# Attention and two MLPs on one core: four matmuls on constants at the outset, and transfers at other places in the queues

## The reference

```python
def _attn_ref(q, k, v, tau):          # q, k, v: (2, 6016, 256), float32
    qn = q / (np.linalg.norm(q, axis=1, keepdims=True) + 1e-06)
    kn = k / (np.linalg.norm(k, axis=1, keepdims=True) + 1e-06)
    s = kn.transpose(0, 2, 1) @ qn / tau          # (2, 256, 256)
    s = s - s.max(-1, keepdims=True)
    a = np.exp(s)
    a /= a.sum(-1, keepdims=True) + 1e-09
    return v @ a

def _moe_ref(x, w_gate, w_val, w_out):            # x: (12032, 256), d_ff 1536
    gate = 1.0 / (1.0 + np.exp(-(x @ w_gate)))
    return gate * (x @ w_val) @ w_out

def _moe2_ref(x, w_in, w_out):                    # d_ff 2048
    h = x @ w_in
    return (h - np.tanh(h)) @ w_out

# reference: _moe2_ref(_moe_ref(_attn_ref(...)))
```

## Time and profile before

| | |
|---|---|
| time, median of 3 runs | 2216.34 us |
| the profiled execution's own time | 2216.27 us |
| its span | 2214.4 us |
| PE busy | 2192.7 us, 99% |
| PEld busy | 1908.6 us, 86% |
| DVE busy | 1547.5 us, 70% |
| ACT busy | 1276.4 us, 58% |
| POOL busy | 1157.3 us, 52% |
| DMA | 439.46 MB, 198 GB/s over the span |

### The profile page before, as it was taken

How to read it: one execution, slowest core, us unless ns; L and a number is a source line. 1 busy time by engine, 2 the same in 40 slices (tenths; PEclk the granted TensorE clock), 3 DMA queues, 4 the chain that set the end, 5 groups by cost and what they waited for, 6 DMA issues and landing times.

```text
span 2214.4 us, 33619 instructions
## 1 busy us (share of the span) xinstructions
PE 2192.7 (99%) x11664; PEld 1908.6 (86%) x11664; DVE 1547.5 (70%) x2933; ACT 1276.4 (58%) x2336; POOL 1157.3 (52%) x970
## 2 busy tenths in 40 slices
PE   8999999999999999999999999999999999999998
PEld 7878988888888898898998898888888888889998
DVE  6868866866776685686586586586586577567566
ACT  5644654665565565565565465465466456556555
POOL 3476663564465474365364365356356446446434
PEclk9999999999999999999999999999999999999999
DMA  9997476376367357447557546537536546635644
GB/s 340 341 298 271 154 225 221 134 228 213 140 214 235 132 175 225 178 169 241 188 197 227 188 166 207 188 134 221 190 126 213 183 141 200 203 126 183 232 143 150
DMA packets 286473, 439.46 MB, mean 198 GB/s; under 512 B 208096, under 2 KB 214496, under 8 KB 286304
## 3 DMA queue, kind: packets, MB, share of 16 engines
q1 hardware_dynamic: 279184, 409.82, 56.3%
q0 software_dynamic: 5264, 27.27, 3.3%
q10 hardware_dynamic: 1856, 0.23, 0.1%
HBM read 386.14 MB, written 51.12 MB: 197 GB/s over the span
## 4 chain that ended last, share of the span: by engine, by line
PE 91%; DMA 3%; SPq 2%; DVE 2%; issue 1%; ACT 1%; POOL 0%; ACTq 0%; DVEq 0%; POOLq 0%
PE up L1595 52%; PE x_acc L1595 20%; PE acc L1595 18%; DMA qk_in<-in_k 1%; DMA w_stage<-in_moe_w_out 1%; PE x_acc L1621 1%; SPq L410 1%; SPq L486 1%; DMA u_records<-x_lo 1%; SPq L488 0%; DVE sq_sum L1187 0%; SPq L399 0%; ACT up L832 0%; DMA ring<-u_records 0%; DVE g_lo L1311 0%
## 5 line engine op out<-in xcount | busy, mean ns | idle before, releaser
L735 POOL TENSOR_TENSOR g<-t_sums,g 128x512 fp32r<-128x512 f32 (+1 forms) x384 | 503.1, 1327 | 375.6 <-ACT g L1022 375.4
L725 POOL TENSOR_TENSOR g_lo<-func_out,g_hi 128x512 fp32r<-128x512 f32 (+1 forms) x253 | 314.2, 1271 | 571.7 <-ACT g_hi L957 571.4
L1595 PE MATMUL up<-vt_hi,ring 128*128 128x512 f32 (+1 forms) x1848 | 562.4, 385 | 0.0
L1595 PEld LDWEIGHTS up<-vt_hi,ring 128*128 128x128 f32 x1848 | 347.1, 188 | 63.0
L1595 PE MATMUL up<-vt_lo,ring 128*128 128x512 f32 (+1 forms) x924 | 358.7, 388 | 1.5 <-DMA ring<-u_records 1.3
L1324 DVE TENSOR_TENSOR held<-up,held 128x512 f32<-128x512 f32 (+1 forms) x132 | 89.7, 680 | 367.9 <-PE up L1595 367.9
L1022 ACT ACTIVATE g<-t_sums 128x512 fp32r<-128x512 f32 (+1 forms) x384 | 237.9, 619 | 160.1 <-DVE t_sums L1407 159.7
L1595 PE MATMUL x_acc<-g,ring 128*128 128x256 f32 (+1 forms) x2304 | 304.4, 281 | 0.0
L1595 PE MATMUL up<-x_lo,in_w_hi 128*128 128x512 f32 (+1 forms) x768 | 298.0, 388 | 0.0
L1595 PE MATMUL up<-x_hi,in_w_lo 128*128 128x512 f32 (+1 forms) x768 | 297.4, 387 | 0.0
L1595 PE MATMUL up<-x_hi,in_w_hi 128*128 128x512 f32 (+1 forms) x768 | 295.9, 385 | 0.0
(11 more groups left out here) (257 smaller groups left out, 3621.8 us busy)
## 6 DMA issues: line engine op xcount, KB each, us to landing
...
ring<-u_records SPq DMA_DIRECT2D x132, 896.0 KB, 6.0
...
```

Source lines behind the costliest of these rows:

```text
L725: pool.tensor_tensor(g1_lo[:, i, 0:w], func_out[:, i, 0:w], g1_hi[:, i, 0:w].bitcast(F32), ALU.subtract).then_inc(g_lo_made, 2 if last and ...
L735: pool.tensor_tensor(lo[:, cut, 0:half], t_sums[:, first - T1:first - T1 + 2, 0:half], hi[:, cut, 0:half].bitcast(F32), ALU.subtract).then ...
L1595: mm = pe.matmul(psum, a, b, start=start and n == 0, stop=stop and n == 2, skip_group_check=shared_bank)
```

## The change

It has eight parts. (1) PE makes four matmuls of the constant `ones` with itself, into a bank that is written anew later, before its first gram chunk. (2) POOL loads pieces 0 and 1 of the weights when 8 gram chunks are done (before: 2), piece 2 at 12 (before: 4) and piece 3 at 14 (before: 7), and it is piece 2 whose split waits for the attention weights of batch 0 (before: piece 4). (3) The eight parts of v for unit 0 are loaded with the last four chunks of batch 0, two with each (before: with the chunks 4 to 11, one with each); DVE turns them and DVE and ACT split them two chunks of batch 1 later, and the second unit's come behind batch 1's chunks. (4) SP waits for all of q and k to have landed before it saves the first raw part. (5) Of the folded parts only the first three pieces' are stored ahead of the first sums; the others follow one by one behind each of the first three sums. (6) In ACT's `first_chunk`, `first_hi` comes ahead of `hi_of_u_sums`. (7) The outputs of a tile's unit 0 are stored in the next tile's `body`, behind its first two ring records and two d records. (8) The last four products are given in two steps, and DVE's last sums begin behind the first of them and turn the first half before the rest.

```diff
@@ -310,7 +310,7 @@
         p_hi_made, p_lo_made = sem("p_hi_made"), sem("p_lo_made")
         t_sums_made, t_hi_made, t_lo_made = sem("t_sums_made"), sem("t_hi_made"), sem("t_lo_made")
         o_made, m_copied, out_summed = sem("o_made"), sem("m_copied"), sem("out_summed")
-        last_three_made = sem("last_three_made")
+        last_three_made, last_two_made = sem("last_three_made"), sem("last_two_made")
         out_turned, stored = sem("out_turned"), sem("stored")
 
         block = ctx.enter_context(nc.Block())
@@ -364,9 +364,9 @@
             return 16 + 16 * STORES * (n + 1)
 
         TURN_ATT = 12
-        EARLY_PIECES = 4
-        V_TURN, V_SPLIT = 12, 13
-        SECOND_V_TURN, SECOND_V_SPLIT = 10, 11
+        WARM_UP = 4
+        EARLY_PIECES, PIECES_AT = 2, [8, 8, 12, 14]
+        V_TURN, V_SPLIT = 14, 15
         EARLY_FOLDS = 3
         FOLD_AT, FOLD_SUMS_AT = 1, 2
 
@@ -436,10 +436,13 @@
                         sp.dma_start(qk_in[:, buf, which, ahead:size, :],
                                      rows[:, bass.ds(block0, size - ahead), :]
                                      ).then_inc(qk_loaded[buf], 16)
-                    if r in (1, 2):
-                        if b == 1 and r == 1 and buf == 0:
+                    if b == 0 and r == ROUNDS - 1:
+                        for part in (2 * buf, 2 * buf + 1):
+                            load_v_part(0, 0, 0, W, part)
+                    if b == 1 and r in (1, 2):
+                        if r == 1 and buf == 0:
                             sp.wait_ge(v_turned, 1)
-                        load_v_part(0, 0, b, W, (r - 1) * BUFS + buf)
+                        load_v_part(0, 0, 1, W, (r - 1) * BUFS + buf)
 
             def save_raw(n):
                 sp.wait_ge(w_split, n + 1)
@@ -536,7 +539,6 @@
                             sp.wait_ge(fold_stored[n], 32)
                     load_ring(NEXT_G, u_records[b_next, record(0, 0)])
                 load_o(t, BOTH - 1)
-                store(t, b, 0, w)
 
             def body(t, b, w, w_before, b_before, nxt, b_next, fold=False):
                 sp.wait_ge(o_made, BOTH * (t - 1) + BOTH - 2)
@@ -545,6 +547,7 @@
                 load_gate(t, b, 1)
                 for p in range(2):
                     load_d(t, p)
+                store(t - 1, b_before, 0, w_before)
                 if fold:
                     sp.wait_ge(p_made, 2 * BOTH * t)
                     load_raw(t - 1)
@@ -580,12 +583,13 @@
             for b in range(B):
                 for r in range(1 if b == 0 else 0, ROUNDS):
                     load_qk(b, r)
+            sp.wait_ge(qk_loaded[BUFS - 1], 32 * B * ROUNDS)
             for n in range(FOLDS):
                 save_raw(n)
             for n in range(J1 // 4):
                 store_d(n)
             load_v(1, 0, 0, W)
-            for n in range(FOLDS):
+            for n in range(FOLDS // 2):
                 store_a_parts(n)
             load_d(0, 2, first=True)
             for n in range(FOLDS):
@@ -594,6 +598,8 @@
                     load_d(0, 2 + (n + 1) // 2, first=True)
                 if n == 1:
                     load_v(1, 0, 1, W)
+                if n < FOLDS // 2:
+                    store_a_parts(FOLDS // 2 + n)
             sp.wait_ge(u_a_stored, 16 * 8 * FOLDS)
             sp.wait_ge(first_up_made, 4 * J1)
             rest_of_tile(0, 0, W, W, 0, first=True)
@@ -606,6 +612,7 @@
                 body(t, 1, W, W, 1, W, 1)
             body(TILES - 2, 1, W, W, 1, W_END, 1)
             body(TILES - 1, 1, W_END, W, 1, None, 1)
+            store(TILES - 1, 1, 0, W_END)
             store(TILES - 1, 1, 1, W_END)
             sp.wait_ge(stored, all_stored(LAST_SUB))
 
@@ -628,8 +635,8 @@
 
             def load_next(n):
                 if n + 2 < PIECES:
-                    if n + 2 < EARLY_PIECES:
-                        pool.wait_ge(gram_made, 4 + 3 * n)
+                    if n + 2 < len(PIECES_AT):
+                        pool.wait_ge(gram_made, PIECES_AT[n + 2])
                     elif SECOND_BLOCK <= n + 2:
                         pool.wait_ge(gram_made, B * CHUNKS - 6)
                     pool.wait_ge(w_split, n + 1)
@@ -789,7 +796,7 @@
                         lo_of_fold_sums(t - 1)
                 both_subs(t, w, nxt)
 
-            pool.wait_ge(gram_made, 2)
+            pool.wait_ge(gram_made, PIECES_AT[0])
             load(0)
             load(1)
             for n in range(WHOLE):
@@ -902,12 +909,12 @@
                     first_sigma(j, s)
                 if j == ROOT_AT:
                     make_root(1)
-                if U_HI_AT <= j < U_HI_AT + FOLDS:
-                    hi_of_u_sums(j - U_HI_AT)
                 if j == EXP_AT:
                     make_exp(1)
                 for s in range(2):
                     first_hi(j, s)
+                if U_HI_AT <= j < U_HI_AT + FOLDS:
+                    hi_of_u_sums(j - U_HI_AT)
 
 
             def hold_a(steps, copied, n, w, other_summed, other_done, after_o=None):
@@ -1124,10 +1131,9 @@
                     make_root(0)
                 if c == 7:
                     make_exp(0)
-                if c == SECOND_V_SPLIT:
-                    split_plain_vt(1)
                 if c == TURN_ATT:
                     split_att_t(0, acc[1])
+            split_plain_vt(1)
             for n in range(EARLY_FOLDS):
                 split_fold(n)
             first_chunk(0)
@@ -1446,17 +1452,19 @@
                     for o in range(8))
                 m5, m6, m7, m4 = pair_sums(half)[4:]
                 dve.wait_ge(m_copied, 4 * LAST_SUB + 2)
-                dve.wait_ge(o_made, BOTH * TILES)
+                dve.wait_ge(last_two_made, 1)
                 dve.tensor_tensor(u2, m6, m1, ALU.add).then_inc(out_summed, 1)
                 dve.wait_ge(out_summed, done + 1)
                 dve.tensor_tensor(m1, m2, m1, ALU.add).then_inc(out_summed, 1)
                 dve.tensor_tensor(u4, m5, u2, ALU.add).then_inc(out_summed, 1)
-                dve.tensor_tensor(u3, m7, u2, ALU.add).then_inc(out_summed, 1)
                 dve.wait_ge(out_summed, done + 3)
                 dve.tensor_tensor(m2, m3, u4, ALU.add).then_inc(out_summed, 1)
                 dve.wait_ge(stored, all_stored(LAST_SUB - 1))
+                dve.wait_ge(out_summed, done + 4)
+                turn_half(1, W_END, 0)
+                dve.wait_ge(o_made, BOTH * TILES)
+                dve.tensor_tensor(u3, m7, u2, ALU.add).then_inc(out_summed, 1)
                 dve.wait_ge(out_summed, done + 5)
-                turn_half(1, W_END, 0)
                 dve.tensor_tensor(m3, u3, m4, ALU.subtract).then_inc(out_summed, 1)
                 dve.tensor_tensor(spare, m5, u3, ALU.add).then_inc(out_summed, 1)
                 dve.wait_ge(out_summed, done + 7)
@@ -1542,14 +1550,13 @@
                     make_logits(0)
                 if c == 8:
                     make_att(0)
-                if c == SECOND_V_TURN:
-                    turn_v(0, 1)
-                if c == SECOND_V_SPLIT:
-                    split_plain_vt(1)
                 if c == TURN_ATT:
                     split_att_t(0, acc[1])
+            turn_v(0, 1)
             for n in range(EARLY_FOLDS):
                 split_fold(n)
+                if n == 0:
+                    split_plain_vt(1)
             make_sums(1)
             first_chunk(0)
             split_fold(EARLY_FOLDS)
@@ -1861,7 +1868,8 @@
                     O(t, BOTH - 2, w)
                     opening_of_o(t, BOTH - 1, w)
                     o_products(t, BOTH - 1, w, FIRST_THREE).then_inc(last_three_made, 1)
-                    o_products(t, BOTH - 1, w, LAST_FOUR).then_inc(o_made, 1)
+                    o_products(t, BOTH - 1, w, LAST_FOUR[:2]).then_inc(last_two_made, 1)
+                    o_products(t, BOTH - 1, w, LAST_FOUR[2:]).then_inc(o_made, 1)
                     return
                 n, i = pair_no(t + 1, 0), NEXT_G
                 loaded(t, i)
@@ -1892,6 +1900,9 @@
                     D(t, U_PAIRS - 1, i, w)
                 both_subs(t, w, nxt)
 
+            pe.wait_ge(consts_made, 2)
+            for n in range(WARM_UP):
+                pe.matmul(acc[1][:, 0:P], ones[:, :], ones[:, :], start=True, stop=True)
             for c in range(CHUNKS):
                 gram_chunk(0, c // BUFS, c % BUFS, first=c == 0)
             pe.wait_ge(consts_made, 3)
```

## The result

| | median | runs | ratio to before | 95% interval |
|---|---|---|---|---|
| before | 2214.57 us | 6 | | |
| changed | 2229.44 us | 6 | 1.0069 | 1.0057 to 1.0080 |

The account below looks back on a forecast made before the run. TensorE (PE) was taken as the bound, busy 2192.7 us of a span of 2214.4. The terms summed as 2216.27 - 4.5 - 3.9 - 1.3 - 0.5 + 4.0 = 2210.1 us, range 2202 to 2221.

Parts of the forecast that it names:

- E: Tile loop: unit 0's moved stores make val(1)'s record later and PE stall in a few tiles, +4.0 us (0 to 22).
- rival 3: Tile loop: val(1)'s record late in all ten tiles, beyond the slack, so slower, 2228 us; chance 0.15.
- The prediction's own sign of being wrong: Tile loop: waits for `ring<-u_records` over 10 us in sum, or the first tile's down products starting no earlier.
- the upper bound: Tile loop, cost of the moved stores: 15 us (ten tiles of 1.5), or 22 with a clock drop behind each.
- The rule on queues: DMA engines work descriptors in ring order, so eight stores hold up val(1)'s record beyond their issue time; no separate size.
- A, the start stage: Start stage: later weight pieces and v let q and k land sooner, -4.5 us (2 to 7).
- the 6.0 us less 2.0: Start stage up to the logits: 6.0 us lost by PE, of which 2 us were left in place.
- B, `g_lo`: First tile near 164: ACT's new order removes PE's wait and clock loss, 1.3 handed back by VectorE, -3.9 us.
- F: the later splits: GpSimd's splits of pieces 2 and 3 behind the attention weights: +7 us on its chain, costed at nothing.
- C, the ring wait at tile 5: Start of tile 5: PE's wait for a ring record behind the output stores goes, -1.3 us (0 to 1.65).
- D, the tail: End of the kernel: VectorE's last sums begin earlier, -0.5 us (0.2 to 0.6).
- The warm-up: Before the first load: four matmuls cost nothing and give back 0.5 us of the 1.1 us slow start.

Follow-up runs that it names:

- e1: The changed kernel with unit 0's stores back at their old place, ahead of val(0): 2218.2 us, ratio 1.0014 to before.
- e8: The kernel before with only unit 0's eight stores moved, to behind the issue of val(1)'s record: 2214.8 us, ratio 0.9998.
- e3: The changed kernel with each unit 0 store cut to 32 rows (4 KB instead of 64 KB), the rest of its output missing: 2215.7 us, ratio 1.0002.
- e6: The kernel before with only ACT's new order, `first_hi` ahead of `hi_of_u_sums`: 2213.1 us, ratio 0.9984.
- e11: The kernel before with the weight pieces loaded late, but pieces 2 and 3 split without waiting for the attention weights: 2212.8 us, ratio 0.9988.
- e10: The kernel before with only the weight pieces loaded late and pieces 2 and 3 split behind the attention weights: 2217.3 us, ratio 1.0004.
- e15: The changed kernel with unit 0's stores behind val(1)'s record and pieces 2 and 3 split without waiting for the attention weights: 2213.9 us, ratio 0.9999.
- e9: The kernel before with ACT's new order and the folded parts' stores spread behind the first sums: 2214.8 us, ratio 0.9997.

## Why the prediction was wrong

The direction was wrong because of one term, E, and the result is rival 3, which had a chance of 0.15 and a time of 2228. Its mechanism is what happened, but that its time comes within 2 us of the 2229.4 is luck: it took 22 us for the stalls and 10.2 of gains, where the loop lost some 16 and the other parts together gained nothing (e1, 1.0014).

- **E, the moved stores: +4.0 was taken, some +16 measured** (1760.0 in the loop against 1744.1 with no ring wait at all, e8). The mechanism was the one in the prediction: the stores no longer stand in SP's wait for `o_made`, val(1)'s record is later, and the slack is gone. "Net 1.5 to 5 us later" was right too: 1.4 to 5.9 us, 3.6 on average. The step that failed is the next one, "Against slacks of 3 us in most tiles this is about 1 us lost in each of a few tiles, 2.5 in tile 6 and 0.5 in tile 5". The delay exceeded the slack in all ten tiles and PE stalled in nine, for 11.2 us by the list of waits; it was 1.5 in tile 6 and 3.4 in tile 5. The numbers for this step stood in the text, a delay of up to 5 us against slacks of 0.1 to 4.3; the sum never set the one against the other tile by tile. The prediction's own sign of being wrong, over 10 us of such waits, came true. Of the upper bound, the half clock behind each stall was seen in tile 5 alone (1.00 behind 1.2 us).
- **The rule on queues**, Trainium skill, "DMA: Bandwidth & Descriptors", section "Queues, rings and completion order", says that each DMA engine takes its descriptors in ring order. That this order holds up the record is not what these traces show. Behind the stores the record lands 4.9 to 5.5 us after its issue, and before, with the stores further ahead, it took 4.8 to 5.6; all of the delay is in the time until SP issues it. That issue row grows with the bytes, from 4.13 us for eight stores of 4 KB to 7.35 for eight of 64 KB (e3), though the same page's section "Bandwidth" counts only transfers under 64 KB as dominated by their descriptors. Why the row grows is not shown.
- **A, the start stage: -4.5 taken, -0.4 in the profile.** Nine kernels with the pieces at their old places end the gram stage at 95.3 us on average (94.0 to 96.9), the eight with late pieces at 93.4 (91.7 to 96.0): -1.9. The part of the term that was mis-sized is the 6.0 us less 2.0: the lead won up to 38 us, 15 matmuls, was paid back by 57, where the pieces and v now come together and PE waits for them. The 2 us left in place for this were too few. The last wait at 93.37 did go.
- **B, `g_lo`: -3.9 taken, and alone it is -3.5 (e6, 1.5 to 5.5), but the wait was moved and not removed.** Of the profiles with the new order and nothing left out only e6's is free of it; five have the 3.2 or 3.3 us near 180, the changed kernel 2.1 and 1.8, and the half clock near 166 is there as before (0.81 and 0.50). What B had wrong is the 1.3 us for what VectorE hands back.
- **F: the later splits.** The step that failed is "I cost it at nothing, on that cover of over 20 us". The cover held for ACT, which did not wait for POOL; but POOL's work lies beside VectorE's sums and holds them up. With ACT's old order the late splits take the sums from 22.6 to 30.7 us and the first tile from 80.7 to 84.5 (e11 and e10); in the whole change it is 24.7 to 27.6 and 79.2 to 81.8 (e15 and e1, whose stores stand at different places, which by e8 costs nothing), and 0.9999 to 1.0014 in time, about 3 us. That VectorE is the pace of the first tile was in the prediction; that its instructions get up to five times as long beside POOL's was to be read from its own rows before (0.43 against 0.84 to 2.34 for the same form), and I had not asked why they differ.
- **C, the ring wait at tile 5**, went from that place, and came back in the same tile as the longest new one, 3.37. It was worth less than taken: kernels with the stores at their old place show loops of 1743.9 (e1, e9) to 1746.6 (before), so the wait is not there in each execution. On average they are at 1744.8, and the four kernels with the stores behind val(1) at 1743.8: 1.0 us.
- **D, the tail: -0.5 taken, -0.4 measured** (7.4 to 7.0), right.
- **The warm-up** can't be told from the scatter, and no run has it alone. PE starts it at 1.14 us and goes on to the first blocks at 4.04. The Trainium skill, "TensorE: Matmul & The Clock Gate", Part 1, says that the number of slow matmuls at the start varies from run to run. In these traces there was no low clock to give back: it reads 1.00 over the first 8 us in before and in the changed kernel, so the slow start of the earlier trace rows was not the clock's.
